# Row additions in halves on GpSimd, a third buffer of token sums, and a new order of work between two expert layers

## The chip, the cores and the metric

The kernel runs on one core of a Trainium2 chip. The metric is the device time of one execution in microseconds (us). Five engines work from queues of their own, each in order: TensorE (PE; its weight loads are PEld), VectorE (DVE), ScalarE (ACT), GpSimd (POOL) and SyncE (SP, which only issues DMAs). They meet at semaphores: an instruction adds to one when it is done, and another engine waits until the count has been reached.

## The reference, cut to what matters

```python
attn = softmax(mask(q k^T / 8)) v              # mask: same cluster of query and key
x = attn as (1536 tokens, 512)
# first layer: each token goes to the one expert of 8 with the largest logit
out[mask] = gate_w[mask] * (relu(x[mask] @ w1[e]) @ w2[e])
# second layer: all 8 experts for all tokens, P from 8 rounds of row and column sums
out += P[:, e:e+1] * (relu(x @ w1[e]) @ w2[e])
```

All in fp32. The kernel writes each fp32 operand as a high part (rounded to the fp32r type of TensorE) and a low part (the rest), and takes three products: high by high, low by high, high by low.

## The kernel before, in words

It has three stages: attention (to about 300 us), the **routed layer** (about 318 to 567 us) and the **dense layer** (to the end). The change touches the second, and the **seam** between it and the third.

**Routed layer.** Tokens are sorted by expert and cut into `ITEMS` = 19 items of up to 128 rows of one expert. For item n TensorE multiplies the rows by w1 in two halves (L1299 to L1301, sources `all_w_*` = w1), transposes the hidden rows (`transpose_h`, L1229), transposes the rows of the next item (L1222) and multiplies by w2 (L1316 to L1318). Both weight matrices are split anew for every item: ScalarE copies the high part (`w1_part`, `w2_part`), VectorE subtracts it to get the low part (`split_lo`, L889), in three parts for w1 and four parts of 128x1024 for w2; `rw2_lo` counts the latter. VectorE's order in item n is: low part of the first half of the hidden (`h_part(n, 0)`, source in PSUM), w2 parts 2 and 3 of n (both sources in SBUF), `h_part(n, 1)`, then for item n+1 w1 part 0, the rows, w1 parts 1 and 2, w2 parts 0 and 1. ScalarE reads the item's result from PSUM times the gate (`read_out`, L1577), and GpSimd adds it to the token rows in `OUT` (`add_rows`, L2281, one 128x512 addition, at once when ScalarE is done; `ry_added` counts). GpSimd also gathers the rows of later items (L2191).

**Token sums.** The dense layer multiplies 2x2 block matrices with seven products instead of eight, and so needs sums of blocks of tokens: for each of 6 pairs of tiles p, four 128x256 results in a buffer `XS` (L2248, L2250, L2258, L2261). Pair p can be formed when item `final(p) - 2` = 13 + p has been added. There are two buffers, used in turn; `transpose_pair(p)` (L1253) sends four blocks m = 0 to 3 through TensorE (`x_t` counts them), ScalarE takes their high parts (`hi_parts(p)`) and VectorE their low parts (`lo_parts(p)`, `x_lo` counts). Block m of pair p waits for `x_lo` of block m of the pair before (the PSUM bank), except for p = 0 and 3.

**Seam.** In the last item (n = 18) the pairs 0, 1, 2 are transposed between its products; `first_unit` is the first unit of the dense layer, with seven products named A11, S1, A12, S2, S3, A22, S4 and the pairs 3, 4, 5 between them. Its intermediate results are copied by ScalarE (`copied` 1, 2, 3 = `CP1`, `CU2`, `CU3`; `CU2` lies on the zero tile of `OUTZ`, so it waits for all additions) and added to by VectorE (`summed`). Product S2 waits for `copied` 1, S3 for `copied` 2, A22 for `copied` 3. The weights of the second unit, (0, 1), need: the load `load1(0, 1)` into `RAW1[1]` (at `scratch_at`), `plain_weights(0, 1)` on ScalarE and VectorE, four sums on GpSimd (`weight_sums(0, 1)`, L2196 to L2201), and `summed_weights(0, 1)` on ScalarE and VectorE. Unit (0, 1) starts with A11, which waits for `x_lo` 21 (the first low part of pair 5), and S1, which waits for `s_lo` 3 (the low part of the summed weights).

In the order before, GpSimd does: add item 17, `next_weight_sums` (sums for the first unit), all sums of pairs 2, 3, 4, add item 18, the last two sums of pair 5 (VectorE has formed the first two, L1888 and L1890), `weight_sums(0, 1)`.

## Time and profile before

| | |
|---|---|
| three runs, median (lowest to highest) | 1592.2 us (1591.24 to 1592.25) |
| the profiled execution | 1594.29 us, its span 1592.5 us |
| mean granted clock of TensorE | 0.995 of full speed |
| busy: PE, PEld | 1568.3 us (98%), 1390.7 us (87%) |
| busy: DVE, ACT, POOL | 1190.0 us (75%), 770.6 us (48%), 263.7 us (17%) |

The span runs from the first to the last instruction. Busy shares are means over the three stages; VectorE for one is busy nearly all the time in the routed layer and far less in the dense one. A number like 562.95 is a moment, in us from the start of the span.

### The profile page before, as it was taken

The numbers are of one execution on the slowest core, as the hardware profiler recorded it, in microseconds if no ns is written. First come the engines' busy times: TensorE is split into PE (matmuls) and PEld (weight loads), VectorE is DVE, ScalarE is ACT, GpSimd is POOL, SyncE is SP. The second block draws the span as 40 slices with busy tenths as digits, with TensorE's granted clock in tenths as the row PEclk, the third lists the DMA queues.
The fourth block names the chain that finished last, engine by engine and source line by source line (L and its number), as shares of the span: only waits on it lengthen the run. The fifth ranks groups of instructions, "written<-read, shape, count | busy, mean of one in ns | idle before, by whom it ended". The sixth has DMA issues, their size and how long they took to land.

```text
span 1592.5 us, 27473 instructions
## 1 busy us (share of the span) xinstructions
PE 1568.3 (98%) x8404; PEld 1390.7 (87%) x8404; DVE 1190.0 (75%) x2026; ACT 770.6 (48%) x1418; POOL 263.7 (17%) x343
## 2 busy tenths in 40 slices
PE   8999999999999999999999999999999999999998
PEld 7999999778888788989999898989899998989897
DVE  7999999999999976876656666666656566666664
ACT  5777779888888852323232323233232333232321
POOL 2111111342333550000100100010001001100102
PEclk9999999999999999999999999999999999999999
DMA  4222323354344310100110010011001100100002
GB/s 101 61 60 69 79 59 90 86 198 148 143 151 151 106 41 27 40 28 27 47 33 27 29 51 27 27 40 40 27 27 45 35 27 28 52 26 27 27 0 79
DMA packets 123701, 94.92 MB, mean 60 GB/s; under 512 B 66345, under 2 KB 101161, under 8 KB 123633
## 3 DMA queue, kind: packets, MB, share of 16 engines
q1 hardware_dynamic: 120848, 86.01, 17.8%
q0 software_dynamic: 2480, 8.13, 1.5%
q8 instruction: 21, 0.34, 0.1%
q14 instruction: 48, 0.39, 0.1%
q10 hardware_dynamic: 304, 0.05, 0.0%
HBM read 87.88 MB, written 6.29 MB: 59 GB/s over the span
## 4 chain that ended last, share of the span: by engine, by line
PE 88%; DVE 7%; issue 3%; ACT 2%; DVEq 0%; DMA 0%; ACTq 0%; POOL 0%
PE moe_bank L1381 11%; PE moe_bank L1383 11%; PE moe_bank L1382 11%; PE moe_bank L1356 10%; PE moe_bank L1359 10%; PE moe_bank L1358 10%; PE attn_ps_out L447 3%; PE attn_ps_probs_t L428 2%; PE moe_bank L1316 2%; PE moe_bank L1318 2%; PE moe_bank L1317 2%; PE moe_bank L1299 2%; PE moe_bank L1301 2%; PE moe_bank L1300 2%; DVE attn_scores L697 1%
## 5 line engine op out<-in xcount | busy, mean ns | idle before, releaser
L2035 DVE SCALAR_TENSOR_TENSOR all_x<-moe_bank,all_x 128x512 f32<-128x512 f32 x336 | 251.4, 749 | 130.8 <-PE moe_bank L1383 130.2
L1356 PE MATMUL moe_bank<-moe_x_t_hi,all_w_hi 128*128 128x384 f32 x896 | 303.0, 338 | 2.0 <-DVE all_w_lo L889 1.4
L1359 PE MATMUL moe_bank<-moe_x_t_hi,all_w_lo 128*128 128x384 f32 x896 | 302.5, 338 | 0.0
L1381 PE MATMUL moe_bank<-moe_w_hi,moe_h_hi 128*128 128x512 f32 x768 | 302.3, 394 | 0.0
L1358 PE MATMUL moe_bank<-moe_x_t_lo,all_w_hi 128*128 128x384 f32 x896 | 301.1, 336 | 0.0
L1382 PE MATMUL moe_bank<-moe_w_lo,moe_h_hi 128*128 128x512 f32 x768 | 300.5, 391 | 0.0
L1383 PE MATMUL moe_bank<-moe_w_hi,moe_h_lo 128*128 128x512 f32 x672 | 264.5, 394 | 0.0
L1356 PEld LDWEIGHTS moe_bank<-moe_x_t_hi,all_w_hi 128*128 128x128 f32 x896 | 168.4, 188 | 13.4 <-issue 2.0
L1358 PEld LDWEIGHTS moe_bank<-moe_x_t_lo,all_w_hi 128*128 128x128 f32 x896 | 168.4, 188 | 10.0
L1359 PEld LDWEIGHTS moe_bank<-moe_x_t_hi,all_w_lo 128*128 128x128 f32 x896 | 168.2, 188 | 0.0
L2196 POOL TENSOR_TENSOR moe_w_sums<-moe_dense_w_raw 128x256 f32<-128x256 f32 x32 | 24.8, 774 | 842.4 <-DVE all_w_lo L889 842.4
L1382 PEld LDWEIGHTS moe_bank<-moe_w_lo,moe_h_hi 128*128 128x128 f32 x768 | 144.1, 188 | 23.0
L1381 PEld LDWEIGHTS moe_bank<-moe_w_hi,moe_h_hi 128*128 128x128 f32 x768 | 144.3, 188 | 21.5
L1383 PEld LDWEIGHTS moe_bank<-moe_w_hi,moe_h_lo 128*128 128x128 f32 x672 | 126.0, 188 | 30.1
L1729 ACT ACTIVATE moe_h_hi<-all_x 128x384 fp32r<-128x384 f32 x63 | 33.1, 525 | 170.4 <-DVE all_x L2147 170.4
L889 DVE TENSOR_TENSOR moe_routed_w_lo<-moe_w_raw,moe_routed_w_hi 128x1024 fp32r<-128x1024 f32 x76 | 112.8, 1524 | 0.1
L1705 ACT ACTIVATE moe_h_hi<-moe_p 128x384 fp32r<-128x384 f32 x63 | 33.1, 525 | 143.2 <-DVE moe_p L2101 143.2
L2101 DVE TENSOR_TENSOR moe_p<-moe_bank,moe_p 128x384 f32<-128x384 f32 x63 | 35.1, 557 | 86.8 <-PE moe_bank L1359 76.1
L643 DVE TENSOR_TENSOR attn_probs_t_lo<-attn_ps_probs_t,attn_probs_t_hi 128x384 fp32r<-128x384 f32 x192 | 97.3, 547 | 2.4 <-ACT attn_probs_t_hi L570 1.3
L1724 ACT ACTIVATE moe_h_hi<-moe_bank 128x384 fp32r<-128x384 f32 x63 | 31.0, 492 | 134.2 <-PE moe_bank L1359 134.2
L697 DVE CUSTOM_DVE_ANT_0 attn_scores<-attn_ps_scores,attn_mask 128x768 f32<-128x768 f32 x96 | 91.2, 950 | 2.5 <-issue 0.6
L564 ACT ACTIVATE attn_probs<-attn_scores,attn_row_max 128x768 f32<-128x768 f32 x96 | 91.4, 952 | 3.4 <-DVE attn_row_max L697 3.3
(339 smaller groups left out, 3071.4 us busy)
## 6 DMA issues: line engine op xcount, KB each, us to landing
all_w_raw<-in_moe_w SPq DMA_DIRECT2D x8, 2048.0 KB, 7.5
moe_w_raw<-in_moe_w SPq DMA_DIRECT2D x8, 2048.0 KB, 8.3
moe_dense_w_raw<-in_moe_w SPq DMA_DIRECT2D x64, 256.0 KB, 2.9
moe_dense_w_raw<-in_moe_w SPq DMA_DIRECT2D x32, 512.0 KB, 3.4
attn_q_raw<-in_q SPq DMA_DIRECT2D x32, 192.0 KB, 3.0
attn_k_raw<-in_k SPq DMA_DIRECT2D x32, 192.0 KB, 3.5
attn_v_raw<-in_v SPq DMA_DIRECT2D x16, 192.0 KB, 3.5
tokens<-all_x SPq DMA_DIRECT2D x32, 96.0 KB, 1.9
```

The costliest lines, as they stand in the source:

```text
L447: mm = pe.matmul(out, V2[j][:, m, :], probs[(s0 // 3) % 2][:, m, :], start=(m == 0 and probs is PTH), stop=(m == T - 1 and probs is PTL))
L564: act.activation(PR[s % 2][:], SM[s % 2][:], ACT.Exp, bias=MX[s % 2][:], scale=-1.0, accum_out=SUM[:, s % 12:s % 12 + 1]).then_inc(exp_don ...
L643: return dve.tensor_tensor(out, src, hi.bitcast(F32), ALU.subtract)
L697: dve.tensor_tensor_reduce(out=SM[s % 2][:].rearrange("p (a k) -> p a k", a=2), in0=ps_s[s % 2][:, :, 0:3 * P], in1=MASK[s % 2][:].rearran ...
L889: return dve.tensor_tensor(out, src, hi.bitcast(F32), ALU.subtract)
L1356: pe.matmul(out, hi[:, s, k, :], XH[chunk][:, x, k, :], start=(start and k == 0), stop=False, skip_group_check=True)
L1358: pe.matmul(out, hi[:, s, k, :], XL[chunk][:, x, k, :], start=False, stop=False, skip_group_check=True)
L1359: mm = pe.matmul(out, lo[:, s, k, :], XH[chunk][:, x, k, :], start=False, stop=(stop and k == 1), skip_group_check=True)
L1381: pe.matmul(out, HH[h][hidden][:, rows], W2H[j][:, f, :], start=(f == 0), stop=False)
L1382: pe.matmul(out, HH[h][hidden][:, rows], W2L[j][:, f, :], start=False, stop=False)
L1383: mm = pe.matmul(out, HL[h][hidden][:, rows], W2H[j][:, f, :], start=False, stop=(f == 1))
L2035: dve.scalar_tensor_tensor(acc, y, PROB[:, row, bass.ds(at, 1)], acc, ALU.mult, ALU.add).then_inc(y_added, 1)
```

## The change

1. `add_rows(n)` becomes two additions of 128x256. The first waits until VectorE has formed w2 parts 0 and 1 of item n+1, the second until it has formed parts 2 and 3; after each of these points VectorE's next operation reads PSUM. The last item's addition has no such waits.
2. A third buffer `token_sums2` at `scratch_at`. The sums of pairs 0, 1, 2 are formed after items 13, 14, 15; those of pairs 3, 4, 5 are placed at the seam. All four sums of pair 5 are now GpSimd's.
3. The buffer lies on `RAW1[1]`, so `load1(0, 1)` waits until pairs 0 to 2 have been transposed (`x_t` 12).
4. In the last item VectorE forms `h_part(n, 0)` ahead of w2 parts 2 and 3. In the first, w2 part 1 of item 1 is formed ahead of the sum of gates.
5. At the seam: GpSimd forms `weight_sums(0, 1)` ahead of the sums of pair 4; ScalarE's `summed_weights(0, 1)` stands ahead of `hi_parts(3)`, VectorE's right behind `CU3`; TensorE transposes pair 5 ahead of product A22.

```diff
+              mem.at("token_sums2", [P, 4, 2 * P], F32, scratch_at)]
+        SUMS_OF_PAIR = [XS[0], XS[1], XS[2], XS[0], XS[1], XS[0]]
+        PAIR_BEFORE = {3: 0, 4: 1, 5: 3}
...
             load2(0, 0)
-            load1(0, 1)
             sp.wait_ge(w1_lo, len(W1_PARTS) * ITEMS)
             load2(0, 1)
+            sp.wait_ge(x_t, 4 * GT)
+            load1(0, 1)
             sp.wait_ge(next_lo, 3)
...
                 multiply(a, 0, 0, S3, T3, False, True).then_inc(chain, 1)
+                transpose_pair(5)
                 pe.wait_ge(copied, 3)
                 multiply(a, 0, 0, A22, T4, False, True).then_inc(chain, 1)
-                transpose_pair(5)
...
                 act.activation(CP1[:], a, ACT.Copy).then_inc(copied, 1)
+                summed_weights(0, 1)
                 hi_parts(3)
...
                 hi_parts(5)
-                summed_weights(0, 1)
...
                 w2_part(1, r, 0)
+                w2_part(1, r, 1)
                 dve.wait_ge(gates_found, 1)
                 dve.tensor_reduce(SCALE[:], ...).then_inc(found, 1)
-                w2_part(1, r, 1)
...
+                h_part(n, 0)
                 w2_part(n, r, 2)
                 w2_part(n, r, 3)
-                h_part(n, 0)
...
                 lo_parts(3)
-                token_sums(5)
                 lo_parts(4)
-                low(0, hh, hl, Q11, CP1[:], 1)
                 dve.wait_ge(cross, 1)
                 dve.wait_ge(copied, 3)
                 dve.tensor_tensor(CU3[:], b, CU3[:], ALU.add).then_inc(summed, 1)
+                summed_weights(0, 1)
+                low(0, hh, hl, Q11, CP1[:], 1)
                 low(0, hh, hl, Q22, CU3[:], 2)
                 low(0, hh, hl, Q21, a, 3)
                 lo_parts(5)
-                summed_weights(0, 1)
...
-                pool.tensor_tensor(OUT[:, bass.ds(t, 1), :].rearrange("p o d -> p (o d)"),
-                                   OUTZ[:, bass.ds(s, 1), :].rearrange("p o d -> p (o d)"), Y[n % 2][:], ALU.add
-                                   ).then_inc(ry_added, 1)
+                for half, (cols, done) in enumerate(((slice(0, D // 2), ry_half), (slice(D // 2, D), ry_added))):
+                    if n + 1 < ITEMS:
+                        pool.wait_ge(rw2_lo, W2_PARTS * (n + 1) + 2 * half + 2)
+                    if half == 1:
+                        pool.wait_ge(ry_half, n + 1)
+                    pool.tensor_tensor(OUT[:, bass.ds(t, 1), cols].rearrange("p o d -> p (o d)"),
+                                       OUTZ[:, bass.ds(s, 1), cols].rearrange("p o d -> p (o d)"), Y[n % 2][:, cols],
+                                       ALU.add).then_inc(done, 1)
...
                 add_rows(n)
-                if n >= ITEMS - 5 and n < ITEMS - 3:
-                    all_token_sums(n - (ITEMS - 5))
+                if ITEMS - 6 <= n < ITEMS - 3:
+                    token_sums(n - (ITEMS - 6))
             add_rows(ITEMS - 2)
             next_weight_sums()
-            all_token_sums(2)
-            all_token_sums(3)
-            all_token_sums(4)
+            token_sums(3)
+            weight_sums(0, 1)
+            token_sums(4)
             add_rows(ITEMS - 1)
             token_sums(5)
-            weight_sums(0, 1)
```

## Rows read from the trace of the kernel before

**Rows 1.** Waits of TensorE, whole span: total us, times, longest us.
```profile
PE moe_bank L1316 <- DVE moe_routed_h_lo L889: 3.3, 4, 1.9
PE moe_bank L1356 <- DVE all_w_lo L889: 1.4, 1, 1.4
PE moe_bank L1356 <- ACT moe_u L1682: 0.6, 1, 0.6
```
**Rows 2.** Windows: us, busy us (instructions) of each engine, TensorE's clock, DMA.
```profile
320.00:500.00 180.00, 179.33 (x881) 145.70 (x880) 172.41 (x153) 155.87 (x187) 58.88 (x39) 1.00 0.46 162
558.00:559.00 1.00, 1.00 (x5) 0.70 (x4) 1.00 (x2) 0.00 (x0) 1.00 (x2) 0.50 0.06 16
```
**Rows 3.** Timeline of VectorE and GpSimd: start, us, instruction, idle before it.
```profile
510.19 3.46 DVE L889 TENSOR_TENSOR moe_routed_w_lo<-moe_w_raw,moe_routed_w_hi 128x1024 fp32r<-128x1024 f32 x2
510.57 1.99 POOL L2281 TENSOR_TENSOR all_x<-all_x,moe_y 128x512 f32 x1 [8.50 <-issue]
512.53 1.72 POOL L2248 TENSOR_TENSOR moe_token_sums<-all_x 128x256 f32<-128x256 f32 x1
...
540.63 2.35 DVE L889 TENSOR_TENSOR moe_routed_w_lo<-moe_w_raw,moe_routed_w_hi 128x1024 fp32r<-128x1024 f32 x2
...
562.57 0.74 POOL L2250 TENSOR_TENSOR moe_token_sums<-all_x 128x256 f32<-128x256 f32 x1
```
**Rows 4.** Timeline of TensorE: first transposes of the hidden rows, items 15 to 18.
```profile
512.23 0.60 PE L1229 MATMUL moe_bank<-all_ident,moe_h_rows 128*128 128x128 f32 x4
...
525.49 0.60 PE L1229 MATMUL moe_bank<-all_ident,moe_h_rows 128*128 128x128 f32 x4
...
538.60 0.60 PE L1229 MATMUL moe_bank<-all_ident,moe_h_rows 128*128 128x128 f32 x4
...
551.07 0.60 PE L1229 MATMUL moe_bank<-all_ident,moe_h_rows 128*128 128x128 f32 x4
```
**Rows 5.** Timelines of VectorE and TensorE in item 1.
```profile
339.17 3.46 DVE L889 TENSOR_TENSOR moe_routed_w_lo<-moe_w_raw,moe_routed_w_hi 128x1024 fp32r<-128x1024 f32 x2
...
343.29 0.50 PE L1316 MATMUL moe_bank<-moe_routed_w_hi,moe_routed_h_hi 128*128 128x512 f32 x1 [0.52 <-DVE moe_routed_h_lo L889]
```
**Rows 6.** Timelines of VectorE and TensorE in the last item.
```profile
549.03 6.80 DVE L889 TENSOR_TENSOR moe_routed_w_lo<-moe_w_raw,moe_routed_w_hi 128x1024 fp32r<-128x1024 f32 x4
...
558.48 1.55 DVE L889 TENSOR_TENSOR all_w_lo<-moe_dense_w_raw,all_w_hi 128x512 fp32r<-128x512 f32 x2
...
556.49 0.50 PE L1316 MATMUL moe_bank<-moe_routed_w_hi,moe_routed_h_hi 128*128 128x512 f32 x1 [1.90 <-DVE moe_routed_h_lo L889]
...
562.95 0.82 PE L1253 MATMUL moe_bank<-all_ident,all_x 128*128 128x128 f32 x6
```
**Rows 7.** A pair of loads into the same kind of buffer (SyncE), and landing times of 12.
```profile
565.11 0.92 SPq L1179 DMA_DIRECT2D moe_dense_w_raw<-in_moe_w  x2
...
DMA to landing us min/median/max: 2.6/3.2/8.6
```
**Rows 8.** Timelines of ScalarE, GpSimd and VectorE at the seam.
```profile
571.14 1.85 ACT L884 ACTIVATE moe_x_t_hi<-moe_bank 128x512 fp32r<-128x512 f32 x4 [2.04 <-PE moe_bank L1253]
...
569.51 2.18 POOL L2281 TENSOR_TENSOR all_x<-all_x,moe_y 128x512 f32 x1 [0.37 <-issue]
...
576.73 1.13 POOL L2197 TENSOR_TENSOR moe_w_sums<-moe_dense_w_raw 128x256 f32<-128x256 f32 x1
...
565.00 2.21 DVE L889 TENSOR_TENSOR moe_x_t_lo<-moe_bank,moe_x_t_hi 128x512 fp32r<-128x512 f32 x4
...
581.49 1.21 DVE L889 TENSOR_TENSOR all_w_lo<-moe_w_sums,all_w_hi 128x1024 fp32r<-128x1024 f32 x1
```
**Rows 9.** Timeline of TensorE at the seam: A11, pair 4, S1 of unit (0, 1).
```profile
567.26 0.44 PE L1356 MATMUL moe_bank<-moe_x_t_hi,all_w_hi 128*128 128x384 f32 x1
...
573.09 0.82 PE L1253 MATMUL moe_bank<-all_ident,all_x 128*128 128x128 f32 x6
...
582.84 0.41 PE L1356 MATMUL moe_bank<-moe_x_t_hi,all_w_hi 128*128 128x384 f32 x1 [1.43 <-DVE all_w_lo L889]
```

More of the change, by code:

```diff
@@ L1006, in expert_layers @@
         XS = [mem.at("token_sums0", [P, 4, 2 * P], F32, scratch_at + 12 * KB),
-              mem.at("token_sums1", [P, 4, 2 * P], F32, scratch_at + 8 * KB)]
+              mem.at("token_sums1", [P, 4, 2 * P], F32, scratch_at + 8 * KB),
+              mem.at("token_sums2", [P, 4, 2 * P], F32, scratch_at)]
+        SUMS_OF_PAIR = [XS[0], XS[1], XS[2], XS[0], XS[1], XS[0]]
+        PAIR_BEFORE = {3: 0, 4: 1, 5: 3}
         pair = [P, 2, D]
@@ L1062, in expert_layers @@
         ry_ready, ry_out, ry_added = mem.sem("routed_y_ready"), mem.sem("routed_y_out"), mem.sem("routed_y_added")
+        ry_half = mem.sem("routed_y_half_added")
         cleared = mem.sem("out_cleared")
@@ L1257, in of @@
                     return [rows[:, k * P:(k + 1) * P] for k in ks]
-                xs = XS[p % 2]
+                xs = SUMS_OF_PAIR[p]
                 pe.wait_ge(ry_added, final(p))
@@ L1879, in h_part @@
                 split_lo(dve, RHL[:, 4 * s:4 * s + 4, :], by_chunk[5 + s], RHH[:, 4 * s:4 * s + 4, :]).then_inc(rh_lo, 1)
-            def token_sums(p):
-                xs = XS[p % 2]
-                dve.wait_ge(ry_added, final(p))
-                if p >= 2:
-                    dve.wait_ge(x_t, 4 * (p - 1))
-                dve.wait_ge(x_sums, 2 * p)
-                dve.tensor_tensor(xs[:, 0, :], OUT[:, p + PAIRS, 0:2 * P], OUT[:, p, 0:2 * P], ALU.subtract
-                                  ).then_inc(x_sums, 1)
-                dve.tensor_tensor(xs[:, 2, :], OUT[:, p + PAIRS, 2 * P:4 * P], OUT[:, p + PAIRS, 0:2 * P], ALU.subtract
-                                  ).then_inc(x_sums, 1)
             def lo_parts(p, first=0, end=4):
@@ L2240, in item_gates_of, with token_sums @@
                                        ).then_inc(item_gates, 1)
-            def all_token_sums(p):
-                xs = XS[p % 2]
+            def token_sums(p):
+                xs = SUMS_OF_PAIR[p]
                 pool.wait_ge(ry_added, final(p))
-                if p >= 2:
-                    pool.wait_ge(x_t, 4 * (p - 1))
+                if p in PAIR_BEFORE:
+                    pool.wait_ge(x_t, 4 * (PAIR_BEFORE[p] + 1))
                 pool.tensor_tensor(xs[:, 0, :], OUT[:, p + PAIRS, 0:2 * P], OUT[:, p, 0:2 * P], ALU.subtract
@@ L2251, in all_token_sums @@
                                    ).then_inc(x_sums, 1)
-                token_sums(p)
-            def token_sums(p):
-                xs = XS[p % 2]
                 pool.wait_ge(x_sums, 2 * p + 1)
```

## The prediction

> **What bounds the kernel now.** I read the page first: TensorE is busy 98% of the span, so only its idle time and its slow time can be won. Next its waits [rows 1], to see where the idle time lies. Of those that the change can reach there are six: four times the w2 products wait for the low part of the hidden (3.3 us, the longest 1.9), once unit (0, 1) waits for its summed weights (1.4), once product A22 of the first unit waits for ScalarE's copy `CU3` (0.6). Then the windows [rows 2]: from 320 to 500 us TensorE is busy 179.3 of 180 us and VectorE 172.4. The routed loop is TensorE's, with VectorE about half a us per item behind it. So relief of VectorE is worth nothing in the plain items, and something only where VectorE is late: item 1, the items with token sums, the last item, and the seam. I read the timelines there [rows 3 to 9].
>
> **Collisions.** Two VectorE operations on w2 take 3.46 us with an addition of GpSimd beside them and 2.35 without; a 128x256 operation of GpSimd takes 1.72 us beside such work and 0.74 alone [rows 3]. So one 128x512 addition costs VectorE 1.1 us, one 128x256 operation half of that, 0.55 us, and GpSimd waits in its turn for the VectorE operation that is running. Beside VectorE's reads of PSUM GpSimd has its short duration.
>
> **Halves, plain items.** VectorE gets 1.1 us back per item. Each half (0.74 us) finds VectorE in a PSUM read (some 0.6 us) or waiting for ScalarE. TensorE sets the period there, so the worth is 0. The second half ends more than half a period later than the whole addition did, and the next gather, queued behind it on GpSimd, is issued that much later; but its rows are wanted only in the second half of the next item, most of a period after that. This also costs 0; if that cover were gone, TensorE would wait in every item.
>
> **Item 1.** TensorE waited 0.52 us for a hidden low part that stood behind two w2 parts lengthened by an addition to 3.46 us [rows 5]. With 2.35 us instead, that wait goes: **0.5 us gained**. The w2 part moved ahead of the sum of gates uses time in which VectorE waited for TensorE; it costs 0.
>
> **Items with sums.** The transposes of rows 4 are 13.26, 13.11 and 12.47 us apart. The last is a plain period, so the two items with sums lost 0.8 + 0.6 = 1.4 us, VectorE being full: an addition (1.1) and two of the four sums (1.1) collide, the other two meet PSUM reads. Afterwards three items have sums, without the addition, but the sums come right behind the second half, beside the w1 low parts, where three or four of them collide: 1.65 to 2.2 us instead of 2.2. VectorE's own work is then 13.2 - 2.2 = 11.0 us, and the period 12.65 to 13.2, a loss of 0.2 to 0.7 in each of three items, 0.6 to 2.1 us. I take 1.2: **0.2 us gained** (bounds 0.7 lost, 0.8 gained).
>
> **Last item.** Four w2 parts took 6.80 us beside GpSimd; alone they would take 2 x 2.35 = 4.7. TensorE stood still for 1.90 us and then ran at a granted clock of 0.50, that is 1.2 GHz, over the window 558 to 559 [rows 2, 6]. With `h_part` first and the sums gone elsewhere TensorE goes on at once. But it is VectorE that ends the item: from 548.9 two w2 parts to 551.2, a wait for ScalarE's high part and `h_part` to 552.7, two parts to 555.1, `lo_parts(0)` 2.2 [rows 8] to 557.3, the plain weights 1.55 plus one collision 0.5 [rows 6] to 559.3, `h_part` to 559.9, first block of `lo_parts(1)` to 560.5. There pair 2 can start. TensorE has been ready since about 558.9: a new stall of some 1.6 us. It starts pair 2 at 560.5 instead of 562.95 [rows 6] and ends it at 562.4; `lo_parts(1)`, the summed weights (1.2) and `lo_parts(2)` (2.2) let A11 start at 565.35 instead of 567.26 [rows 9]. **At this point 1.9 us have been gained** (the 0.2 is in it). The slow clock was hidden in the same way: VectorE's low parts of pair 2 ended only just before 567.26.
>
> **Seam.** Now the moved load counts. It was early and free; it now waits for pair 2, 562.5. A pair of loads takes 0.92 us to issue and each some 3.2 us to land [rows 7]; the same pair issued at 565.11 would be down about 3.3 us later, so `RAW1[1]` is there at **565.8**. Queued behind that wait on SyncE are only loads that are needed later. Queued behind it on ScalarE (`plain_weights(0, 1)`) are the second weights, the read-out of item 18 and `CP1`, about 2.9 us, until 568.7: S2 needs `CP1` at 570.1, so there is cover of 1.4 us. On GpSimd everything else stands behind it: `weight_sums(0, 1)` (now ahead of pair 4), the sums of pair 4, the addition of item 18, pair 5. Four sums take 2.8 us alone and 5.8 us if VectorE meets them all (rows 3); one of the same group took 1.13 us [rows 8]. VectorE works on plain and second weights in that time, so I take 4.5: to 570.3. ScalarE, with `summed_weights(0, 1)` ahead of `hi_parts(3)`, splits to 571.4; first block of pair 3 high (0.5) and low (0.6) to **572.5**. Only then may pair 4 be transposed. It was at 573.09 before [rows 9], so the 1.9 us have shrunk to 0.6, and TensorE has stood still for some 1.5 to 2 us.
>
> From there: sums of pair 4 to 573.2; addition of item 18 in two halves without waits, 1.6 against 2.18 [rows 8], to 574.8; on ScalarE `CU2`, `hi_parts(4)` (1.85) and `CU3` to 577.5; on VectorE low parts of pair 4 and `CU3` to 578.6, summed weights 1.2 to 579.8, three low parts of the hidden 1.6 and a collision to 581.8, first block of pair 5 to 582.4. Unit (0, 1) starts there with A11 and comes to S1, 1.05 us later, at **583.5** against 582.84 [rows 9]. The 1.43 us wait for summed weights is gone, but one for pair 5 has taken its place: a loss of 0.7 us.
>
> The first two sums of pair 5 leave VectorE and cost GpSimd 2 x 0.74 us. The Trainium skill (Perfetto Trace Analysis, Optimizing GPSIMD Operations) says to prefer other engines where possible; here it speaks against part 2 of the change, and by it those 1.5 us of GpSimd's queue would be saved. Pair 5 is wanted by TensorE at about 577 and has its sums at 577.7, so the sum above would not change: that chain ends ahead of the one through VectorE.
>
> **Sum.** -0.5 (item 1) + 0.7 (seam, with all that lies between) = +0.2 us. It is made against the profiled execution (1594.29 us), 2.1 us above the median of the three runs; the difference carries over, so 1592.2 + 0.2 = **1592.4 us**.
>
> **Rivals.** *Forecast*, no change that can be told (0.2% is 3.2 us, about what a measurement of this kernel can tell): 0.62.
> *GpSimd's chain does not bind.* If the load lands 1 us sooner and the four sums meet little (2.8 us), the seam chain is 2.7 us shorter; the 1.9 us stay, and the waits of 1.4 and 0.6 us [rows 1] go too: 0.5 + 1.9 + 1.4 + 0.6 = 4.4, so 1587.8. For it: GpSimd's chain has no other fixed point. Against it: VectorE has two plain and one second split in exactly that time. 0.12.
> *GpSimd's chain is longer: slower.* Place: the wait for `RAW1[1]`. The four weight sums all collide (5.8, +1.3), so do those of pair 4 (+2), the landing takes 4 us (+0.8): 4.1 more, 1596.5. It decides against the kernel as soon as the weight sums end later than about 573, since every us after that goes into the start of unit (0, 1) one to one. 0.15.
> *The clock falls at the new stall.* After 1.9 us of standing still TensorE ran at 1.2 GHz [rows 2, 6]; a stall of about the same length is now ahead of pair 4. It would add up to 1.8 us, half of some 3.6 us of slow work, of which the idle time ahead of unit (0, 1) hides most; 1593.9 if it hides little. 0.06. The Trainium skill (TensorE: Matmul & The Clock Gate, HAM oscillation) tells the same mechanism, gaps that bring the clock down again and again; by it the sum would get this term at the seam, and the trace agrees in the last item.
> *The halves do not do what they say.* They still meet VectorE's SBUF work, as the waits order only their start: then item 1 keeps its 0.5 us and nothing else changes, 1592.9. 0.05.
>
> **Range.** The forecast's own bounds: items with sums -0.6 to +0.9, load and weight sums -1.5 to +1.3, clock 0 to +1.5, which gives 1590.1 to 1595. To leave no more than 2 in 10 out I go a little toward both other cases: **1589.3 to 1595.9**. Faster by over 0.2% (below 1589.0) 0.12; slower (above 1595.4) 0.16; the same 0.72.
>
> **What would show it.** Plain periods of 12.4 to 12.5 us, w2 pairs at 2.35 us and halves at 0.74. The wait in item 1 and the 1.9 us one gone, a new one of 1 to 2 us ahead of pair 2, A11 some 2 us earlier. `load1(0, 1)` issued behind pair 2, ScalarE and GpSimd idle until it lands; a TensorE wait of 1.5 to 2 us ahead of pair 4, another ahead of unit (0, 1). I am wrong if pair 4 starts right behind S2, or if the weight sums end before 569 or after 573.

## The result, and the profile after

| | before | changed |
|---|---|---|
| median of 5 runs (lowest to highest) | 1592.25 us (1591.24 to 1593.16) | 1606.47 us (1605.25 to 1607.26) |
| ratio (95% interval) | 1 | 1.009 (1.0076 to 1.0104) |
| the profiled execution, its span | 1594.29 us, 1592.5 us | 1605.63 us, 1603.8 us |
| mean granted clock of TensorE | 0.995 | 0.993 |

The change costs 14.2 us by the medians. The prediction, 1592.4 us with a range to 1595.9, was wrong. The two profiled executions differ by 11.3 us only (before's lay 2.0 above its median, the changed kernel's 0.8 below), and the traces explain those 11.3.

The waits of TensorE from item 1 to the second layer of the dense stage, of the changed kernel; of before it is [rows 1] (us in total, times, longest):

```profile
PE moe_bank L1227 <- DMA moe_x_rows<-tokens,moe_token_of_item: 8.5, 2, 5.4
PE moe_bank L1258 <- DVE moe_x_t_lo L889: 3.1, 2, 2.3
PE moe_bank L1361 <- DVE moe_x_t_lo L889: 1.2, 1, 1.2
PE moe_bank L1361 <- ACT all_x L1685: 0.4, 1, 0.4
```

The waits for low parts of the hidden (3.3 us) and for the summed weights (1.4 us) are gone, as forecast. A wait that the forecast does not have leads the list: twice, 8.5 us in all, TensorE waits for the rows of a coming item, that is for the gather on GpSimd. The timeline of GpSimd in the changed kernel, around the first of the two (start, us, instruction, idle time before it and what ended that):

```profile
503.07 0.74 POOL L2273 TENSOR_TENSOR all_x<-all_x,moe_y 128x256 f32 x1 [3.25 <-DVE moe_routed_w_lo L889]
503.89 1.78 POOL L2240 TENSOR_TENSOR moe_token_sums<-all_x 128x256 f32<-128x256 f32 x1
505.63 1.78 POOL L2242 TENSOR_TENSOR moe_token_sums<-all_x 128x256 f32<-128x256 f32 x1
507.36 2.78 POOL L2245 TENSOR_TENSOR moe_token_sums<-all_x,moe_token_sums 128x256 f32<-128x256 f32 x1
510.22 1.60 POOL L2248 TENSOR_TENSOR moe_token_sums<-all_x,moe_token_sums 128x256 f32<-128x256 f32 x1
511.97 1.77 POOL L2183 DMA_INDIRECT moe_x_rows<-tokens,moe_token_of_item  x1
```

The second half of item 13's addition waits for VectorE's w2 parts; the four sums behind it all collide (1.60 to 2.78 us instead of 0.74); only then does the gather of item 16's rows leave, at 511.97. TensorE's timeline shows when they are wanted, and when they come:

```profile
511.11 0.60 PE L1234 MATMUL moe_bank<-all_ident,moe_h_rows 128*128 128x128 f32 x4
...
518.52 1.11 PE L1227 MATMUL moe_bank<-all_ident,moe_x_rows 128*128 128x128 f32 x4 [5.41 <-DMA moe_x_rows<-tokens,moe_token_of_item]
...
548.40 0.65 PE L1227 MATMUL moe_bank<-all_ident,moe_x_rows 128*128 128x128 f32 x4 [3.13 <-DMA moe_x_rows<-tokens,moe_token_of_item]
```

They are wanted at 513.1 (518.52 less the wait of 5.41), 1.1 us after the issue. The same happens once more at 548.40, to the rows of item 18, behind the sums formed after item 15 (gather issued at 544.14). The sums after item 14 meet nothing, since VectorE was idle by then for want of rows, so the gather between is in time. The windows of the changed kernel add what such a stall costs afterwards (us; busy us and instructions of PE, PEld, DVE, ACT, POOL; TensorE's clock; DMA share, GB/s):

```profile
511.00:514.00 3.00, 2.11 (x12) 1.40 (x10) 3.00 (x4) 2.82 (x4) 2.83 (x3) 1.00 0.92 306
514.00:517.00 3.00, 0.00 (x0) 0.00 (x0) 2.60 (x2) 0.00 (x0) 1.70 (x2) 0.67 1.02 412
517.00:520.00 3.00, 1.48 (x6) 1.39 (x7) 0.00 (x0) 0.33 (x1) 2.84 (x5) 0.50 0.55 201
520.00:523.00 3.00, 3.00 (x13) 2.46 (x12) 0.57 (x1) 1.47 (x3) 1.49 (x2) 0.69 0.99 335
549.00:552.00 3.00, 3.00 (x11) 2.45 (x10) 0.33 (x1) 1.56 (x3) 0.72 (x1) 0.53 0.00 0
```

The clock goes from 1.00 to 0.50 (1.2 GHz) during the stall and is back at 1.00 some 3 to 4 us after work has begun again. The second row also shows the DMA engines busy throughout, mostly with the weight loads that are under way beside the gather. Its median time from issue to landing is 6.2 us from 480 to 600 us.

**Where the 11.3 us are.** I split each trace at three moments of TensorE: the first transposes of token rows ("routed start", 317.47 us in before, 316.94 in the changed kernel), A11, and the first product of the second layer of the dense stage, with `moe_h_hi` as source (585.02 and 596.38 us; it is the first product with a w2 there). From that last moment to the end the two kernels are alike: 1592.5 - 585.02 = 1007.5 and 1603.8 - 596.38 = 1007.4 us. So everything lies in the two pieces between.

| piece of the profiled execution | before | changed | |
|---|---|---|---|
| routed start to A11 | 249.79 | 257.74 | +8.0 |
| A11 to the second layer ("seam piece") | 17.76 | 21.70 | +3.9 |

In the first piece the transposes of the hidden rows [rows 4] tell more. Against before, measured from the start of the span, item 15's are 1.1 us early in the changed kernel (511.11 against 512.23), item 16's 5.2 us late, item 17's 4.7, item 18's 9.6, A11 7.4. So the first gather cost 6.3 us (5.4 of it waiting), the second 4.9 (3.1 of it waiting), and the last item gave 2.2 back. What the slow clock has in the two rests, beside other losses, I did not separate. The seam piece is GpSimd's and ScalarE's queue behind the late load, in the changed kernel (timelines of GpSimd, ScalarE and TensorE, and one window):

```profile
576.00 0.75 POOL L2188 TENSOR_TENSOR moe_w_sums<-moe_dense_w_raw 128x256 f32<-128x256 f32 x1 [2.90 <-DMA moe_dense_w_raw<-in_moe_w]
...
580.53 1.06 ACT L884 ACTIVATE all_w_hi<-moe_w_sums 128x1024 fp32r<-128x1024 f32 x1 [1.73 <-POOL moe_w_sums L2193]
...
582.95 1.19 PE L1258 MATMUL moe_bank<-all_ident,all_x 128*128 128x128 f32 x6 [2.28 <-DVE moe_x_t_lo L889]
...
586.25 0.64 PE L1361 MATMUL moe_bank<-moe_x_t_hi,all_w_hi 128*128 128x384 f32 x1 [0.41 <-ACT all_x L1685]
...
593.14 0.45 PE L1361 MATMUL moe_bank<-moe_x_t_hi,all_w_hi 128*128 128x384 f32 x1 [1.24 <-DVE moe_x_t_lo L889]
```

```profile
584.00:586.00 2.00, 1.84 (x9) 1.44 (x8) 0.32 (x1) 0.29 (x1) 1.70 (x3) 0.50 0.00 0
```

GpSimd waits 2.90 us for the load, forms the weight sums until 580.5, ScalarE splits them, and pair 4 is transposed 2.28 us late; behind that TensorE runs at 1.2 GHz (the window, at 0.50), and waits again ahead of S3 (for `CU2`, at 586.25) and of A11 of unit (0, 1) (for the first low part of pair 5, at 593.14).

### The profile page after: what moved, and what is told of

Same layout as the page of the kernel before. It is cut to its first block, busy times and chain, and to the rows that moved or that the text cites. A ratio compares the mean times of both kernels' runs of the same rounds, so it can differ in the third digit from the quotient of the medians.

```text
span 1603.8 us, 27528 instructions
## 1 busy us (share of the span) xinstructions
PE 1572.2 (98%) x8404; PEld 1392.8 (87%) x8404; DVE 1173.7 (73%) x2024; ACT 771.1 (48%) x1418; POOL 260.9 (16%) x364
## 4 chain that ended last, share of the span: by engine, by line
PE 85%; DVE 6%; issue 3%; POOL 1%; ACT 1%; DMA 1%; DVEq 0%; ACTq 0%; POOLq 0%; SPq 0%
PE moe_bank L1386 11%; PE moe_bank L1388 11%; PE moe_bank L1387 11%; PE moe_bank L1361 10%; PE moe_bank L1364 10%; PE moe_bank L1363 10%; PE attn_ps_out L447 2%; PE moe_bank L1321 2%; PE attn_ps_probs_t L428 2%; PE moe_bank L1323 2%; PE moe_bank L1322 2%; PE moe_bank L1304 2%; PE moe_bank L1306 2%; PE moe_bank L1305 2%; DVE attn_scores L697 1%
## 5 line engine op out<-in xcount | busy, mean ns | idle before, releaser
L889 DVE TENSOR_TENSOR moe_routed_w_lo<-moe_w_raw,moe_routed_w_hi 128x1024 fp32r<-128x1024 f32 x76 | 94.0, 1276 | 0.1
```

The lines of the kernel that those rows point to most:

```text
L889: return dve.tensor_tensor(out, src, hi.bitcast(F32), ALU.subtract)
```

## The experiments

Each run gave a median against before's, run on the same chip beside it, and a profile that I split as above. Theory G: the gathers behind the halves and the sums make the loss of the routed layer. Theory S: the late load together with the new order makes the loss of the seam.

| kernel | median, before beside it | ratio (95%) | to A11 | seam piece |
|---|---|---|---|---|
| before | | | 249.79 | 17.76 |
| changed | 1606.47, 1592.25 | 1.009 (1.0076 to 1.0104) | 257.74 | 21.70 |
| e1_gather_first | 1596.27, 1593.15 | 1.0023 (1.0013 to 1.0033) | 248.73 | 21.89 |
| e2_whole_additions | 1595.61, 1593.15 | 1.0017 (1.0008 to 1.0027) | 248.60 | 20.84 |
| e3_halves_alone | 1593.39, 1593.15 | 1.0001 (0.9991 to 1.0011) | 250.06 | 18.90 |
| e4_old_seam_order | 1603.04, 1593.15 | 1.0061 (1.0044 to 1.0078) | 257.62 | 18.47 |
| e5_gather_first_old_seam | 1594.19, 1593.37 | 1.0004 (0.9996 to 1.0013) | 248.78 | 20.05 |
| e6_load_late_alone | 1593.62, 1593.37 | 1.0002 (0.9993 to 1.0012) | 249.59 | 17.76 |
| e7_before_gather_first | 1591.07, 1593.37 | 0.9991 (0.9983 to 1.0000) | 249.16 | 17.73 |
| e8_new_order_alone | 1594.54, 1593.37 | 1.0011 (1.0002 to 1.0020) | 248.51 | 18.57 |
| e9_gather_first_new_seam | 1593.23, 1593.25 | 1.0000 (0.9990 to 1.0010) | 249.11 | 19.04 |
| e10_new_order_late_load | 1595.68, 1593.25 | 1.0018 (1.0009 to 1.0027) | 249.56 | 22.92 |
| e11_halves_gather_first | 1592.87, 1593.25 | 0.9999 (0.9990 to 1.0008) | 247.88 | 18.37 |
| e12_new_seam_low_part_first | 1592.10, 1593.25 | 0.9995 (0.9986 to 1.0004) | 248.15 | 18.05 |

The last two columns are from one execution each, the medians from 4 (e4) to 12.

**The clock in the column "to A11".** From item 18's first transposes of the hidden rows to A11, six kernels have the last item of before, with its wait of 1.86 to 1.90 us. In five of them (before, e6, e7, e9, e10) the clock falls behind that wait and the stretch takes 16.17 to 16.19 us. In e8_new_order_alone, which has changed nothing by that point, the clock stays at 1.00 behind a wait of 1.89 us, and the stretch takes 15.02 us (its timeline of TensorE and a window, to be set beside [rows 2] and [rows 6]):

```profile
556.03 0.50 PE L1316 MATMUL moe_bank<-moe_routed_w_hi,moe_routed_h_hi 128*128 128x512 f32 x1 [1.89 <-DVE moe_routed_h_lo L889]
```

```profile
558.00:560.00 2.00, 2.00 (x19) 1.91 (x17) 2.00 (x4) 1.84 (x5) 1.92 (x3) 1.00 0.04 8
```

So 1.2 us of any lead over before at A11 can be the slow clock of before's one profiled execution. The same stretch takes 15.04 and 15.03 us with `h_part(n, 0)` first and whole additions (e2, e12), 14.14 and 14.28 with halves and the old order in the last item (e3, e11), and 14.03 or 14.04 with both (the changed kernel, e1, e4, e5).

### The changed kernel with the gathers ahead of the sums

```diff
                 gather(n + 2)
-                add_rows(n)
-                if ITEMS - 6 <= n < ITEMS - 3:
-                    token_sums(n - (ITEMS - 6))
+                if ITEMS - 6 < n <= ITEMS - 3:
+                    token_sums(n - 1 - (ITEMS - 6))
+                add_rows(n)
```

> The changed kernel, but GpSimd issues the gather of item n+2 ahead of the token sums of items 13 to 15 instead of behind them. Theory G (the gathers of items 16 and 18 come late because they stand behind a late second half and four colliding sums): the two waits of TensorE for gathered rows (5.4 and 3.1 us) go, and the 1.2 GHz stretches behind them; 9 to 11 us back, near 1596 us, with the seam's loss left. Rival S (the loss is mostly the seam's: load, weight sums and clock): under 5 us back, above 1601. Rival L (the gathers are late because the weight loads fill the DMA engines, whatever their place in the queue): the waits shrink by less than half, 1602 or more.

Measured: 10.2 us less than the changed kernel, 11.1 if each is taken against before beside it (+3.1, where the changed kernel had +14.2). No wait for rows is left from item 1 on, and A11 comes at 248.73, 9.0 us earlier than in the changed kernel and 1.06 ahead of before, which is no more than before's slow clock in the last item. GpSimd's timeline in this kernel, to be set beside the one above:

```profile
502.45 0.75 POOL L2273 TENSOR_TENSOR all_x<-all_x,moe_y 128x256 f32 x1 [3.25 <-DVE moe_routed_w_lo L889]
503.35 1.94 POOL L2183 DMA_INDIRECT moe_x_rows<-tokens,moe_token_of_item  x1
505.31 1.79 POOL L2240 TENSOR_TENSOR moe_token_sums<-all_x 128x256 f32<-128x256 f32 x1
```

The gather leaves 8.6 us earlier (8.0 measured from item 14's first transposes of the hidden rows), though the halves and their waits are as they were. Theory G holds for the routed layer; the rival that the weight loads make the gathers late whatever their place in the queue fails. The seam piece keeps its whole loss (21.89), so it is not a consequence of the gathers. Nor is it one of the slow clock: here the clock stays at 1.00 through the seam, behind an even longer wait ahead of pair 4 (timeline of TensorE, and a window).

```profile
573.45 0.85 PE L1258 MATMUL moe_bank<-all_ident,all_x 128*128 128x128 f32 x6 [2.45 <-DVE moe_x_t_lo L889]
```

```profile
574.00:576.00 2.00, 1.46 (x11) 0.89 (x9) 0.83 (x2) 0.24 (x1) 1.33 (x2) 1.00 0.00 0
```

### The changed kernel with whole additions

```diff
-                for half, (cols, done) in enumerate(((slice(0, D // 2), ry_half), (slice(D // 2, D), ry_added))):
...
+                pool.tensor_tensor(OUT[:, bass.ds(t, 1), :].rearrange("p o d -> p (o d)"),
+                                   OUTZ[:, bass.ds(s, 1), :].rearrange("p o d -> p (o d)"), Y[n % 2][:], ALU.add
+                                   ).then_inc(ry_added, 1)
```

> The changed kernel with the old whole addition, issued as soon as the result is there; sums still ahead of the gather, seam unchanged. Theory G says that the second half's wait is what made the gather late: without it the gather is issued about 5 us earlier and TensorE waits for no rows; the 0.5 us of item 1 is lost again; the last item is somewhat later. About 1597 us. If the colliding sums alone made it late (rival C), a wait for rows of 1 us or more stays in items 15 and 17 and the time is above 1600.

Measured: the waits for rows are gone here as well. The sums still collide, in this kernel's timeline of GpSimd:

```profile
498.11 1.61 POOL L2240 TENSOR_TENSOR moe_token_sums<-all_x 128x256 f32<-128x256 f32 x1
499.68 1.79 POOL L2242 TENSOR_TENSOR moe_token_sums<-all_x 128x256 f32<-128x256 f32 x1
501.44 1.72 POOL L2245 TENSOR_TENSOR moe_token_sums<-all_x,moe_token_sums 128x256 f32<-128x256 f32 x1
503.24 1.65 POOL L2248 TENSOR_TENSOR moe_token_sums<-all_x,moe_token_sums 128x256 f32<-128x256 f32 x1
505.04 1.82 POOL L2183 DMA_INDIRECT moe_x_rows<-tokens,moe_token_of_item  x1
```

They take 6.8 us and the gather is in time. So the collisions of the sums alone do not make it late; it takes the second half's wait. The sums start 0.4 us behind item 14's first transposes of the hidden rows here (498.11 - 497.72), and 5.3 us behind them in the changed kernel (503.89 - 498.56).

### The kernel before with the halves alone

```diff
-                pool.tensor_tensor(OUT[:, bass.ds(t, 1), :].rearrange("p o d -> p (o d)"),
...
+                for half, (cols, done) in enumerate(((slice(0, D // 2), ry_half), (slice(D // 2, D), ry_added))):
```

> The kernel before with part 1 of the change alone (additions in halves with their waits); two buffers, sums after items 14 and 15, old seam. Theory G: one gather (item 18's, behind the sums of pair 1) or both come late, as in the changed kernel, since the sums stand behind the second half here too: 2 to 8 us slower, 1594 to 1600. Rival: the halves cost nothing and the third buffer with its third set of sums does it: within 1 us of the kernel before, or 1 us faster.

Measured: no difference (1.0001), where 2 to 8 us had been expected; by the time alone the rival would hold. The trace has the forecast wait all the same, and what cancels it. TensorE waits once for rows in this kernel:

```profile
PE moe_bank L1223 <- DMA moe_x_rows<-tokens,moe_token_of_item: 2.1, 1, 2.1
```

Its gather was issued 12.3 us behind item 15's first transposes of the hidden rows (522.12 - 509.80), against 6.2 in before (518.44 - 512.23). Item 18 begins its transposes 2.3 us late against before, from the routed start, and the stretch from there to A11 is 2.05 us shorter. The waits for low parts of the hidden fell from 3.3 to 0.3 us. Even alone, halves and sums use up the cover of the gather.

### The changed kernel with the old order at the seam

Late load, halves and third buffer stay; the orders of TensorE, ScalarE, VectorE and GpSimd at the seam are those of before.

```diff
-            weight_sums(0, 1)
             token_sums(4)
             add_rows(ITEMS - 1)
             token_sums(5)
+            weight_sums(0, 1)
```

> The changed kernel with the order of the kernel before at the seam (weight sums last, ScalarE and VectorE take them last, pair 5 behind A22, VectorE forms its first two sums); halves, third buffer, late load and late gathers stay. If the new order costs (GpSimd's weight sums wait for the load and hold up ScalarE and so pair 4): 3 to 4 us back, 1602 to 1603 us, and no wait above 0.5 us ahead of pair 4. If it is the late load itself that costs, 1 us or less comes back, 1605 or more.

Measured: 3.4 us less than the changed kernel, 4.3 if each is taken against before beside it (+9.9 and +14.2). In the profiled execution 3.2 us are in the seam piece (18.47 against 21.70), with the waits for rows nearly unchanged (8.3 us).

### Both together: gathers ahead of the sums, old order at the seam

The two edits above in one kernel.

> The changed kernel with both cures: gather ahead of the sums, and the old order at the seam. If the two losses are separate and add up (9 to 10 us for the gathers, 3.4 for the order), this takes 1606.5 - 10.2 - 3.4 = about 1592.5 us or a little less, 0 to 2 us under the kernel before, with no wait of TensorE above 1.6 us. If they overlap, it stays at 1594.5 or more.

Measured: 1.0004, so with both causes out the rest of the change is worth nothing measurable; the gain of 0 to 2 us over before that had been expected is not there (+0.8 by the medians). A11 is 1.0 us ahead of before, but the seam piece is 20.05. Its waits there are short, and yet the clock falls; two lines of this kernel's timeline of TensorE, two of its windows:

```profile
579.51 0.44 PE L1361 MATMUL moe_bank<-moe_x_t_hi,all_w_hi 128*128 128x384 f32 x1 [0.50 <-DVE moe_x_t_lo L889]
582.26 0.59 PE L1361 MATMUL moe_bank<-moe_x_t_hi,all_w_hi 128*128 128x384 f32 x1 [1.44 <-DVE all_w_lo L889]
```

```profile
582.00:584.00 2.00, 1.74 (x6) 1.77 (x7) 1.41 (x3) 0.91 (x2) 1.74 (x3) 0.58 0.32 72
584.00:586.00 2.00, 2.00 (x9) 2.00 (x8) 0.10 (x1) 0.00 (x0) 1.41 (x2) 0.56 0.65 190
```

In before no wait stood so close ahead of the one of 1.43 us [rows 9], and the clock stayed at 1.00. But two waits close together are not enough to make it fall. e4_old_seam_order has the same pair (its timeline of TensorE), e11_halves_gather_first too (0.51 and 1.43 us), and in both the clock stayed at 1.00; their seam pieces are 18.47 and 18.37, so the slow clock cost some 1.6 us in this execution.

```profile
589.56 0.44 PE L1361 MATMUL moe_bank<-moe_x_t_hi,all_w_hi 128*128 128x384 f32 x1 [0.52 <-DVE moe_x_t_lo L889]
592.31 0.41 PE L1361 MATMUL moe_bank<-moe_x_t_hi,all_w_hi 128*128 128x384 f32 x1 [1.43 <-DVE all_w_lo L889]
```

### The kernel before with the late load alone

```diff
             load2(0, 0)
-            load1(0, 1)
             sp.wait_ge(w1_lo, len(W1_PARTS) * ITEMS)
             load2(0, 1)
+            sp.wait_ge(x_t, 4 * GT)
+            load1(0, 1)
```

> The kernel before with one edit: the load of the second unit's weights waits until pair 2 has been transposed. If the late load costs by itself, ScalarE's copy for product S2 comes late: 1 to 3 us slower. If it costs only together with the new order (weight sums ahead of pair 4, ScalarE waiting for them ahead of pair 3), it is hidden here: within 0.5 us of the kernel before.

Measured: 1.0002, the seam piece 17.76 as in before. In the old order nothing on the path waits for that load.

### The kernel before with the gathers ahead of the sums

The edit of the first experiment, on the kernel before.

> The kernel before with one edit: the gather ahead of the token sums. There the gathers landed in time, so the gather itself gives nothing; but the sums move by some 2 us against VectorE's work. Within 1 us of the kernel before, 1 us faster at best. A control for the first experiment: if this gained several us, the reading of that one would be wrong.

Measured: 0.9991 (0.9983 to 1.0000), the lowest ratio of all (2.3 us by the medians, more than the 1 us that had been allowed). A11 and the second layer come 0.6 us earlier after the routed start. The interval touches 1; I do not call it faster.

### The kernel before with the new order alone, then with the late load as well

```diff
                 act.activation(CP1[:], a, ACT.Copy).then_inc(copied, 1)
+                summed_weights(0, 1)
                 hi_parts(3)
...
                 hi_parts(5)
-                summed_weights(0, 1)
...
+            weight_sums(0, 1)
             all_token_sums(4)
             add_rows(ITEMS - 1)
-            token_sums(5)
-            weight_sums(0, 1)
+            all_token_sums(5)
```

The lines of VectorE and TensorE that are moved as in the change are left out here; the second kernel has the edit of the late load as well.

> The kernel before with the new order at the seam alone (weight sums ahead of pair 4 on GpSimd, summed weights early on ScalarE and VectorE, pair 5 ahead of A22, all sums of pair 5 on GpSimd), load early, two buffers. If the order costs only because the load is late: within 1 us of the kernel before, the 1.4 us wait for the summed weights replaced by one for pair 5. If the order costs by itself: 3 us slower or more.

> The kernel before with the new order at the seam and the load of RAW1[1] behind the transposes of pair 2; two buffers, whole additions, gathers as before. The new order alone gave +1.2 us and the late load alone +0.3 us. Theory 'order and load cost only together' (the weight sums now stand ahead of pair 4's and must wait for the load, so pair 4, its transposes and everything in VectorE's queue behind the low part of the summed weights come late): a wait of GpSimd for the load of 1.5 to 3 us ahead of the weight sums, TensorE waits 1.5 to 3 us in two or three places between A11 and S1 of unit (0, 1), first product of the second layer at 269.5 to 271 us after the routed start (before 267.55), median 2 to 4 us over before's. Rival 'the seam's loss in the changed kernel comes from its late gathers or its colliding halves': no more than the sum of the two, +1.5 us or less.

Measured: +1.2 us for the order, +2.4 with the late load, where the load alone had +0.25. The mechanism of the second kernel is the forecast's: GpSimd waits for the load, and TensorE ahead of pair 4 (timelines of GpSimd and TensorE, a window):

```profile
567.76 0.75 POOL L2196 TENSOR_TENSOR moe_w_sums<-moe_dense_w_raw 128x256 f32<-128x256 f32 x1 [3.06 <-DMA moe_dense_w_raw<-in_moe_w]
...
574.70 0.85 PE L1254 MATMUL moe_bank<-all_ident,all_x 128*128 128x128 f32 x6 [2.45 <-DVE moe_x_t_lo L889]
```

```profile
578.00:580.00 2.00, 2.00 (x8) 1.90 (x8) 1.93 (x4) 1.37 (x5) 1.89 (x3) 0.50 0.00 0
```

With the load early, the list of waits has 1.2 us for the low part of pair 5 and 0.9 for `CU2`, and none ahead of pair 4 for a low part. Theory S holds in its mechanism. In size, the profiled execution shows a seam piece longer by 5.2 us, but it was the slowest of the eleven (1598.43 us), with the clock below 1.00 from 576 to 584; the median says that the two together cost 2.4 us, of which some 1 us (2.4 - 1.2 - 0.25) is the interaction. The intervals are about 1.4 us to each side, so that last figure is uncertain. Traces with the clock at 1.00 through the seam give more: with the new order, 18.57 with the load early (e8) and 20.84 or 21.89 with it late (e2, e1), though these two differ from e8 in more than the load.

### Three attempts at a faster kernel

The first takes the gathers ahead of the sums on the kernel before and places the weight work of unit (0, 1) otherwise; the second is the halves with the gathers ahead; the third is the first with `h_part(n, 0)` first in the last item.

```diff
             all_token_sums(4)
+            weight_sums(0, 1)
             add_rows(ITEMS - 1)
             token_sums(5)
-            weight_sums(0, 1)
...
                 act.activation(CU3[:], a, ACT.Copy).then_inc(copied, 1)
+                summed_weights(0, 1)
                 act.wait_ge(summed, 2)
...
-                lo_parts(5)
+                lo_parts(5, 0, 2)
                 summed_weights(0, 1)
+                lo_parts(5, 2, 4)
```

> The kernel before with the gathers ahead of the token sums, and with the second unit's weight work placed differently: GpSimd forms weight_sums(0, 1) behind the sums of pair 4 and ahead of the last addition, ScalarE copies their high part behind the copy to CU3, VectorE their low part between the second and third low part of pair 5. Load early, two buffers, whole additions. Theory 'the seam only has to keep S1 of unit (0, 1) supplied': the wait of 1.43 us ahead of that S1 goes and nothing takes its place; with the 0.66 us from the gathers the first product of the second layer comes 1.5 to 2.5 us earlier after the routed start than in the kernel before (267.55 us there), so 265.0 to 266.0, and the median is 1.5 to 2.5 us under before's. Rival 'any wait removed here comes back a few products on' (the high parts of pair 5 are now late by 0.94 us of ScalarE's copy): the first product of the second layer at 266.7 to 267.2, median within 0.8 us of before's.

> The kernel before with the additions in halves and the gathers ahead of the token sums, nothing else. Halves alone gave +0.02 us with one wait for rows of 2.1 us. Theory 'the halves themselves help and only their effect on the gather hurts': no wait for rows, the waits of TensorE for low parts of the hidden rows (3.3 us in before) down to under 2 us, first product of the second layer at 266 to 267 us, median 1 to 2 us under before's. Rival 'the halves are worth nothing in themselves': median as with the gathers alone moved, 0.5 to 1.5 us under before's and not under that kernel's, first product at 266.9 us.

> The kernel before with the gathers ahead of the sums, the placement of the second unit's weight work as in the run before last of this set that has it (weight sums behind pair 4's sums), and in the last item the low part of the hidden rows ahead of the low parts of w2. Theory 'the last item's gain is its own': A11 is 1.3 to 2.2 us earlier after the routed start than in the kernel before (249.79), and the gain stays up to the second layer if pair 4's sums and the weights are in time: first product of the second layer at 263.5 to 265 us, median 2.5 to 4 us under before's. Rival 'GpSimd's chain at the seam sets the end there, so an earlier A11 is given back as a wait': A11 earlier by the same 1.3 to 2.2 us, first product of the second layer within 0.5 us of the kernel with the same seam and the old order in the last item.

Measured: 1.0000, 0.9999 and 0.9995. All three missed what was expected of the median. In the first the 1.43 us wait is gone, and the second layer comes later all the same (249.11 + 19.04 = 268.15 against 267.55). The third has the same seam with the clock at 1.00 and takes 18.05, so the slow clock is 1.0 us of it; but 18.05 is no less than the 17.76 of before either, so the wait that was removed came back in others. The first two rows are windows of the first of the three kernels, the last two of the third:

```profile
574.00:576.00 2.00, 1.20 (x7) 0.87 (x6) 1.75 (x4) 2.00 (x6) 1.28 (x2) 1.00 0.00 0
576.00:578.00 2.00, 2.00 (x7) 1.90 (x8) 1.41 (x4) 1.32 (x2) 0.00 (x0) 0.54 0.00 0
```

```profile
574.00:576.00 2.00, 1.19 (x7) 0.87 (x6) 2.00 (x5) 2.00 (x5) 0.81 (x2) 1.00 0.00 0
576.00:578.00 2.00, 2.00 (x18) 1.97 (x17) 1.41 (x3) 1.36 (x4) 0.00 (x0) 1.00 0.03 8
```

Both kernels have the same two waits of TensorE ahead of these windows, 0.91 and 0.81 us; in one execution the clock falls to 0.54, in the other it stays at 1.00. In the second kernel A11 comes at 247.88 against 249.16 with the gathers alone, and the seam gives 0.6 of that back; of the 1.28 us, 1.2 are the clock, which fell in the last item of the one and not of the other. In the third, A11 is 1.6 us ahead of before and the second layer 1.35 (266.20 against 267.55); the rival of that expectation, which allows it no more than 0.5 us over the kernel with the old last item, cannot be judged directly, since that kernel's trace had the slow clock twice. Taking 1.2 and 1.0 us for it off 268.15 gives an estimate of 266.0, and this speaks for the rival. No version beats before by more than the measurement can tell.

## Why the prediction was wrong

**Halves, plain items: right in the routed loop.** From 340 to 500 us TensorE is busy 160.00 of 160 us, each half takes 0.74 us and two w2 parts 2.35. The worth is 0, as said.

**The cover of the gather: the step that failed.** The step compared the delay of the gather with its cover for plain items only, and carried the answer, 0, to the items with sums without working it out there. There four sums stand between the second half and the gather. One line of before's timeline of GpSimd, right behind those of [rows 3], would have told it:

```profile
518.44 1.82 POOL L2191 DMA_INDIRECT moe_x_rows<-tokens,moe_token_of_item  x1 [0.15 <-issue]
```

The period has a fixed point, the first transposes of the hidden rows. The next item's rows are wanted 14.5 us behind it (513.1 - 498.6 in the changed kernel, the latter one plain period of 12.5 us ahead of 511.11). Before issued its gather behind sums 6.2 us after that point (518.44 - 512.23) and its gathers took 4.5 us to land in the median, so 14.5 - 6.2 - 4.5 = 3.8 us of cover were left. That is less than the half period of 6.2 us by which the step itself let the second half end later. In the changed kernel the gather was issued 511.97 - 498.6 = 13.4 us after the point. Of the 7.2 us more, the sums took 2.1 to 2.2 (7.9 us from 503.89 instead of 5.8), and the second half's wait the other 5. The loss of 11.2 us (6.3 + 4.9) in the routed layer comes from here: with the sums behind the gather A11 comes 9.0 us earlier, with whole additions 9.1, and by the medians, each against before beside it, they gave back 11.1 and 11.8 us.

**Item 1: right.** The 0.52 us wait [rows 5] is gone; TensorE is busy 179.84 of the 180 us from 320 on, against 179.33 [rows 2].

**Items with sums: the collisions right, their place in the queue not costed.** "Three or four of the sums collide" came true (1.60 to 2.78 us each). I charged them to VectorE's period alone, and not to what stands behind them on GpSimd. By 511.11 the changed kernel is 1.1 us ahead of before, 0.5 of it from the attention stage, so VectorE's side was not where the large loss lay. But the forecast's 0.2 us gained is not borne out either. The changed kernel cannot show it, as VectorE catches up while TensorE waits for rows; in e1_gather_first, without those waits, the transposes of rows 4 are 13.59, 13.59 and 12.99 us apart, and from 0.7 us ahead of before at item 14 it falls to 1.1 us behind at item 18, both counted from the routed start: a loss of 1.8 us. There the sums stand ahead of the addition, a turn later.

**Last item: the number right, half of it for another reason.** 1.9 us had been forecast up to A11, 0.2 of it from the items with sums, so 1.7 from the item itself; it gave 2.2 (9.6 us late at item 18's first transposes, 7.4 at A11). The new wait ahead of pair 2 was forecast at 1.6 us and is 0.78. The prediction held that before's slow clock was hidden there; e8_new_order_alone, with the same wait and the clock at 1.00, reaches A11 1.17 us sooner, so it was not, and 1.2 of the 2.2 us are clock that before does not lose in every execution. The other 1.0 us comes with the halves: `h_part(n, 0)` first with whole additions takes as long as e8's old last item (15.03 and 15.02 us), halves with the old order 14.14. So the 0.96 us by which the third attempt's A11 is ahead of the first's is the clock too.

**Seam: the mechanism right, the size too small.** Forecast: pair 4 late by 1.5 to 2 us, then unit (0, 1) late, 2.6 us lost after A11 (1.9 gained there, 0.7 lost at S1). Measured: pair 4 waits 2.28, S3 0.41, A11 of unit (0, 1) 1.24, and the piece is 3.9 us longer. The weight sums took 4.5 us, as forecast. The mis-sized term is the arrival of the load: at its issue, 572.11, and landing, 575.96, it is there 1.28 us after A11, where the forecast had 0.45 (3.85 us from issue to landing against 3.3, the rest a later issue). That makes 0.8 of the 1.1 us by which pair 4 is later than forecast (8.27 us after A11 instead of 7.15). The clock, at 0.50 over 584 to 586, which I had as a rival and gave 0.06, fell but cost nothing here: from pair 4's first transposes to A11 of unit (0, 1) the changed kernel takes 10.19 us and e1_gather_first, at 1.00, 10.20, with 1.21 us of waiting ahead of S3 where the changed kernel has 0.41. So the argument that the idle time behind it hides the slow clock was right for the changed kernel; in e10_new_order_late_load, where the slow clock lasted until 584, the same stretch took 11.24. The Trainium skill (TensorE: Matmul & The Clock Gate, HAM oscillation) tells of gaps that bring the clock down again and again; the trace of the changed kernel agrees in three places, the two waits for rows and the one ahead of pair 4, but e8_new_order_alone (1.89 us) and e1_gather_first (2.45 us) have gaps of that kind with the clock at 1.00.

**The 1.5 us of GpSimd for pair 5's first sums: right, they hide.** Pair 5's blocks wait 0.31 us for a sum in the changed kernel, no more. The Trainium skill, cited there (Perfetto Trace Analysis, Optimizing GPSIMD Operations), advises against compute on GpSimd because the engine is generally slower. The sums after items 13 and 15 did cost here, but for another reason: what stood behind them in its queue was late (the gather, issued at 511.97).

**The rivals and the range.** None of them had the place. "GpSimd's chain is longer" had the engine, at the seam; what decided lay 60 us earlier in the same engine's queue. The bounds that the prediction lists for its range add up to 1590.3 and 1596.1 us, not 1590.1 and 1595; the measured time is outside either way.

## What to carry to other kernels

When an engine that issues DMAs also computes, every wait or longer operation put ahead of the issue is paid out of the DMA's cover; work out that cover (moment wanted, minus moment issued, minus landing) at the tightest place of the loop, not in the plain iteration. And where two edits touch the same resource, one that makes it late and one that puts more behind it, cost them together: the late load and the new order cost +0.25 and +1.2 us alone and +2.4 together, and undoing the order alone gave 3.2 us back in the seam piece of the changed kernel. The halves and the sums are the other pair: the sums behind whole additions left the gather in time, behind halves they did not.

## What the runs showed of the hardware

**The same waits of TensorE bring its clock down in one execution and not in another.** In the last item a wait of 1.86 to 1.90 us was followed by 0.50 (1.2 GHz) in five profiled executions and by 1.00 in a sixth (e8). Waits of 2.28 and 2.45 us ahead of pair 4 were followed by 0.50 in the changed kernel and in e10, and one of 2.45 us by 1.00 in e1. Waits of 0.50 and 1.44 us, 2.75 us from start to start, were followed by 0.58 and 0.56 over four us in e5, and the same pair by 1.00 in e4 and e11. Waits of 0.91 and 0.81 us were followed by 0.54 in e9 and by 1.00 in e12. A wait of 1.43 us with none within 2.75 us ahead of it was not followed by a fall in any of the three traces that have it (before, e6, e7). What decides between the two is not known from these runs. Where nothing behind it hid the slow clock, it cost 1.0 to 1.6 us (last item 16.19 against 15.02, seam of e5 against e4 20.05 against 18.47, of e9 against e12 19.04 against 18.05).

**The clock goes with most of the scatter.** Of 33 runs of the kernel before beside the last four experiments, the 3 with a mean clock of 0.998 took 1590.74 to 1590.98 us, the 6 with 0.994 took 1594.73 to 1595.22. So a single execution cannot settle 2 us.

**A GpSimd operation can be held for as long as the VectorE operation beside it.** 128x256 took 0.74 us alone, 1.6 to 1.8 beside 128x1024 work of VectorE and 2.78 beside its 128x2048 low part, which took 2.83 us itself (2.28 us elsewhere).

**The gathers took longer to land in the changed kernel.** From 480 to 600 us their median from issue to landing is 6.2 us in the changed kernel, with 412 GB/s moving from 514 to 517, where TensorE waited for one, against 4.5 in before. That the loads are the reason was not tried.
